# Linear attention before two MLPs: scores and state product in four array tiles of 64 by 64, half of the late scores left out

## What is computed

```python
f = 1.0 / (1.0 + np.exp(-f_logit))
for t in range(S):
    state = f[:, :, t, :, None] * state + np.einsum('bhd,bhe->bhde', k[:, :, t], v[:, :, t])
    y[:, :, t] = np.einsum('bhd,bhde->bhe', q[:, :, t], state)
...
xn = x / rms * rms_g
g = xn @ w_gate
silu = g * (1.0 / (1.0 + np.exp(-g)))
val = xn @ w_val
return (silu * val @ w_out).astype(np.float32)
...
h = x @ w_in
g = np.where(pos, h, np.where(neg, 0.0, (h + beta) ** 2 / (4.0 * beta)))
return (g @ w_out).astype(np.float32)
```

## Time and profile before

| | |
|---|---|
| time, median of 3 runs | 977.84 us (976.65 to 978.01) |
| the profiled execution's own time | 976.92 us |
| its span, first to last instruction | 975.2 us |
| PE busy | 959.0 us (98%), 7651 matmul records |
| DVE busy | 573.8 us (59%) |
| ACT busy | 326.1 us (33%) |
| POOL busy | 22.5 us |
| DMA engines | 12.6% of their time |
| clock granted to PE | 1.0, in all 40 slices |

### The profile page before, as it was taken

One profiled execution on the slowest core, in us unless ns is written; L12 is line 12 of the kernel. 1 busy time (PEld: TensorE's weight loads), 2 busy tenths in 40 slices (PEclk: granted clock), 3 DMA queues, 4 the chain that ended last, 5 costly groups with the idle time before them and its releaser, 6 DMA issues.

```text
span 975.2 us, 19135 instructions
## 1 busy us (share of the span) xinstructions
PE 959.0 (98%) x7651; PEld 868.6 (89%) x7651; DVE 573.8 (59%) x1098; ACT 326.1 (33%) x556; POOL 22.5 (2%) x58
## 2 busy tenths in 40 slices
PE   6899999999999999999999999999999999999998
PEld 5899999999999999999999998888888888888886
DVE  8788666565674765765664665545545455445443
ACT  2433322322322322223223453333333343333333
POOL 0100000000000000000000000000000000000000
PEclk9999999999999999999999999999999999999999
DMA  5541111011111120210111310000000000000000
GB/s 195 181 161 43 41 42 50 32 48 40 40 40 40 40 73 8 72 41 21 60 40 49 122 57 1 1 33 0 0 32 0 0 32 0 32 0 0 32 1 33
DMA packets 16766, 42.32 MB, mean 43 GB/s; under 512 B 1376, under 2 KB 7648, under 8 KB 16736
## 3 DMA queue, kind: packets, MB, share of 16 engines
q1 hardware_dynamic: 16736, 41.88, 12.6%
HBM read 37.16 MB, written 4.72 MB: 43 GB/s over the span
## 4 chain that ended last, share of the span: by engine, by line
PE 94%; DVE 3%; issue 1%; POOL 0%; ACT 0%; DMA 0%; DVEq 0%; POOLq 0%
PE gate_ps L416 15%; PE val_ps L416 15%; PE acc L492 13%; PE gate_ps L480 10%; PE val_ps L480 10%; PE acc L438 10%; PE acc L496 7%; PE acc L442 5%; PE tb L327 2%; PE y_ps L351 2%; PE y_ps L357 2%; PE tb L337 1%; DVE qd L738 1%; PE ta L313 1%; DVE after L717 1%
## 5 line engine op out<-in xcount | busy, mean ns | idle before, releaser
L658 ACT ACTIVATE raw<-raw,half_col 128x512 f32<-128x512 f32 x96 | 69.4, 722 | 155.3 <-DVE raw L909 155.3
L492 PE MATMUL acc<-high,low 128*128 128x512 f32 x285 | 110.9, 389 | 0.0
L492 PE MATMUL acc<-high 128*128 128x512 f32 x285 | 110.9, 389 | 0.0
L597 ACT ACTIVATE act_buf<-gate_ps 128x384 f32<-128x384 f32 x96 | 47.2, 492 | 177.1 <-PE gate_ps L416 177.1
L602 ACT ACTIVATE high<-h_buf 128x384 fp32r<-128x384 f32 x96 | 50.5, 526 | 167.2 <-DVE h_buf L849 167.2
L416 PE MATMUL gate_ps<-high 128*128 (+1 forms) x288 | 99.3, 345 | 1.0 <-issue 0.6
L438 PE MATMUL acc<-high 128*128 128x384 f32 x288 | 99.1, 344 | 0.0
L416 PE MATMUL val_ps<-high 128*128 (+1 forms) x288 | 99.1, 344 | 0.0
L416 PE MATMUL gate_ps<-high,low 128*128 (+1 forms) x288 | 96.5, 335 | 0.0
L416 PE MATMUL val_ps<-high,low 128*128 (+1 forms) x288 | 96.4, 335 | 0.0
L416 PE MATMUL gate_ps<-low,high 128*128 (+1 forms) x288 | 96.4, 335 | 0.0
(11 more groups left out here) (119 smaller groups left out, 1906.8 us busy)
## 6 DMA issues: line engine op xcount, KB each, us to landing
raw<-qkf_dram SPq DMA_DIRECT2D x21, 768.0 KB, 4.3
x_all<-wb_dram SPq DMA_DIRECT2D x12, 576.0 KB, 5.0
v_sb<-v_dram SPq DMA_DIRECT2D x24, 192.0 KB, 2.8
out_dram<-x_all SPq DMA_DIRECT2D x5, 768.0 KB, 3.8
raw<-wc_dram SPq DMA_DIRECT2D x7, 384.0 KB, 3.1
x_all<-qkf_dram SPq DMA_DIRECT2D x2, 768.0 KB, 6.5
kd<-wc_dram SPq DMA_DIRECT2D x3, 384.0 KB, 2.9
qd<-wc_dram SPq DMA_DIRECT2D x3, 384.0 KB, 3.6
```

Of the source, the lines that this page charges most:

```text
L492: pe.matmul(acc[:, m, 0:N2], wc_part(w, j, 1, m), h2_hi[:, j % 2, :], start=(j == 0 and w is w_hi), stop=False)
L658: nc.scalar.activation(act2_buf[:, j % 2, :], act2_buf[:, j % 2, :], ACT.Square, bias=half_col[:, :], scale=0.5).then_inc(square_ready, 1)
```

## The change

- The scores go in four array tiles of 64 rows by 64 columns: for each pair two halves `h` of the keys and two heads `r`. From the fourth chunk on the later 64 keys are multiplied only with the later 64 queries. So that both halves of the array's columns get as much to do, the two key halves stand swapped in the odd pairs (`decay_k` writes them so, in two instructions; `v` comes swapped from the host; the mask has a second form).
- The state product (`recall`) goes in four tiles of 64 by 64 too, one head each, and the state shrinks from 96 to 48 columns. It now stands ahead of `update`, for all four pairs at once, and the values part (`attend`) behind it, also for all pairs.
- `update` goes in strips of 32 and 16 columns, four side by side, the same tiling as `attend`.
- `y_ps` becomes two banks, one for each `r`, and the second is shared with `ta`; the first three chunks use two banks of `acc`. `turn_kd` of later chunks waits for `xs_ready`. In `first_attention` `turn_kd` of the next chunk comes behind the whole `attend`.
- The semaphore `y_made` rises once in a chunk in place of twice, and the weights of the first MLP are reordered on the host to the new order of heads.

```diff
@@ the state, the mask and the banks
-        state = sb("state", [P, 2, NP, 2 * D])
-        decayed = sb("decayed", [P, NP, 2 * D])
+        state = sb("state", [P, 2, NP, D])
+        decayed = sb("decayed", [P, NP, D])
-        causal = sb("causal", [P, C])
+        causal = sb("causal", [P, 2, C])
-        y_ps = bank("y_ps")
-        ta = bank("ta")
+        y_ps = ctx.enter_context(nc.psum_tensor("y_ps", [P, 2, 512], F32))
         tb = bank("tb")
+        ta = y_ps[:, 1, :]
+        y_first = acc[:, 1:3, :]
@@ PE
                 def turn_kd(n, c):
                     pe.wait_ge(kd_ready, n + 1)
-                    if not isinstance(n, int) or n > 0:
+                    if not isinstance(n, int) or n >= CT:
+                        pe.wait_ge(xs_ready, n)
+                    elif n > 0:
                         pe.wait_ge(scores_ready, 2 * n)
...
                     pe.wait_ge(kdT_ready, n + 1)
+                    pe.sem_inc(score_begun, 1)
                     for p in range(NP):
-                        for r, t in enumerate((tb, ta)):
-                            rows = slice(r * HP, (r + 1) * HP)
-                            mm = pe.matmul(t[:, p * C:(p + 1) * C], kd[rows, c % 2, p, :], qd[rows, c % 2, p, :],
-                                           start=True, stop=True)
+                        for h in range(2):
+                            t0 = HP if not first and h != p % 2 else 0
+                            for r, t in enumerate((tb, ta)):
+                                rows = slice(r * HP, (r + 1) * HP)
+                                mm = pe.matmul(t[h * HP:(h + 1) * HP, p * C + t0:(p + 1) * C],
+                                               kd[rows, c % 2, p, h * HP:(h + 1) * HP],
+                                               qd[rows, c % 2, p, t0:C], start=True, stop=True)
                     mm.then_inc(scores_made, 1)
+
+                def recall(n, c, y):
+                    pe.wait_ge(scores_ready, n * 2 + 2)
+                    pe.wait_ge(decayed_ready, n + 1)
+                    if not isinstance(n, int) or n > 0:
+                        pe.wait_ge(xs_ready, n)
+                    pe.sem_inc(recall_begun, 1)
+                    for p in range(NP):
+                        for h in range(2):
+                            q = slice(h * HP, (h + 1) * HP)
+                            for r in range(2):
+                                rows = slice(r * HP, (r + 1) * HP)
+                                pe.matmul(y[q, r, p * D:(p + 1) * D], qd[rows, c % 2, p, q], decayed[rows, p, :],
+                                          start=(p == 0), stop=False, skip_group_check=True)
@@ update(n)
                         for r in range(2):
-                            mm = pe.matmul(tb[r * HP:r * HP + D, p * D:(p + 1) * D], kdT[:, p, r * HP:r * HP + D],
-                                           v_sb[:, r, p, :], start=True, stop=True)
+                            for d0, d1 in ((0, QW), (QW, D)):
+                                rows = slice(r * HP + d0, r * HP + d1)
+                                mm = pe.matmul(tb[rows, p * D:(p + 1) * D], kdT[:, p, rows],
+                                               v_sb[:, r, p, :], start=True, stop=True)
@@ attend
...
+                def attend(n, y):
+                    for p in range(NP):
                         for r in range(2):
                             for s in range(C // QW):
                                 q = slice(s * QW, (s + 1) * QW)
+                                mm = pe.matmul(y[q, r, p * D:(p + 1) * D], scores[:, r, p, q], v_sb[:, r, p, :],
                                                start=False, stop=True, skip_group_check=True)
@@ slot o == 9, and the first chunks
+                            recall(n, c, y_ps)
                             update(n)
-                            attend(n, c, 0)
-                            attend(n, c, 1)
+                            attend(n, y_ps)
...
+                        recall(n, n, y_first)
                         update(n)
-                        attend(n, n, 0)
+                        attend(n, y_first)
                         if n + 1 < CT:
                             turn_kd(n + 1, n + 1)
-                        attend(n, n, 1)
-                        if n + 1 < CT:
                             score(n + 1, n + 1, True)
@@ DVE: decay_k, decay_state, mask_scores
-                    nc.vector.tensor_tensor(kd[:, c % 2, :, :], raw[:, 1, :, :], after[:, :, :], ALU.mult)\
-                        .then_inc(kd_ready, 1)
+                    nc.vector.tensor_tensor(kd[:, c % 2, 0::2, :], raw[:, 1, 0::2, :], after[:, 0::2, :], ALU.mult)
+                    turned, k_odd, after_odd = (x.rearrange("d a (h t) -> d a h t", h=2) for x in
+                                                (kd[:, c % 2, 1::2, :], raw[:, 1, 1::2, :], after[:, 1::2, :]))
+                    nc.vector.tensor_tensor(turned[:, :, ::-1, :], k_odd, after_odd, ALU.mult).then_inc(kd_ready, 1)
...
-                                            whole[:, c % 2, :].unsqueeze(2).to_broadcast([P, NP, 2 * D]), ALU.mult)\
+                                            whole[:, c % 2, :].unsqueeze(2).to_broadcast([P, NP, D]), ALU.mult)\
...
-                                            causal[:, :].unsqueeze(1).to_broadcast([P, NP, C]), ALU.mult)\
+                                            causal[:, :, :].rearrange("p b t -> p (b t)").unsqueeze(1)
+                                            .to_broadcast([P, NP // 2, 2 * C]), ALU.mult)\
```

More of the change, by code:

```diff
@@ L60, with build @@
 SMALLEST = 2.0 ** -60
-def build(nc, qkf, v, rms_g, wb, wc, out, y_rows):
+def build(nc, qkf, v, v_rows, rms_g, wb, wc, out, y_rows):
     ctx = ExitStack()
@@ L157, in build @@
         kdT_ready = sem("kdT_ready")
+        score_begun = sem("score_begun")
+        recall_begun = sem("recall_begun")
         scores_made = sem("scores_made")
@@ L296, in _ @@
                                         base=0, pattern=[[-1, P]], channel_multiplier=1).then_inc(consts_ready, 1)
+                for h in range(2):
+                    rows = slice(h * HP, (h + 1) * HP)
+                    pool.wait_ge(consts_ready, 6 + h)
+                    nc.gpsimd.affine_select(out=causal[rows, 1, :], in_=causal[rows, 1, :], compare_op=ALU.is_ge,
+                                            fill=0.0, base=(h - 1) * HP, pattern=[[1, C]],
+                                            channel_multiplier=-1).then_inc(consts_ready, 1)
                 with pool.Fori(0, NCH) as n:
@@ L387, in keep_warm @@
                     for _ in range(count):
-                        pe.matmul(acc[:, 0, 0:P], ident[:, :], causal[:, :], start=True, stop=True)
+                        pe.matmul(acc[:, 0, 0:P], ident[:, :], causal[:, 0, :], start=True, stop=True)
                 def first_attention():
@@ L778, in update_state, with normalise @@
                     for r in range(2):
-                        rows, cols = slice(r * HP, r * HP + D), slice(r * D, (r + 1) * D)
-                        ins = nc.vector.tensor_tensor(state[rows, 1, :, cols], u[rows, :, :],
-                                                      decayed[rows, :, cols], ALU.add)
+                        rows = slice(r * HP, r * HP + D)
+                        ins = nc.vector.tensor_tensor(state[rows, 1, :, :], u[rows, :, :],
+                                                      decayed[rows, :, :], ALU.add)
                     ins.then_inc(state_ready, 1)
-                def normalise(n):
+                def normalise(n, y=y_ps):
                     dve.wait_ge(rstd_ready, n + 1)
-                    nc.vector.scalar_tensor_tensor(out=xs[:, :], in0=y_ps[:, 0:DM], scalar=rstd[:, :],
-                                                   in1=g_rows[:, :], op0=ALU.mult, op1=ALU.mult)\
+                    heads = [x[:, :].rearrange("t (r m) -> t r m", r=2) for x in (xs, g_rows)]
+                    nc.vector.scalar_tensor_tensor(out=heads[0], in0=y[:, :, 0:NP * D], scalar=rstd[:, :],
+                                                   in1=heads[1], op0=ALU.mult, op1=ALU.mult)\
                         .then_inc(xs_ready, 1)
@@ L957, in _ @@
                         dve.wait_ge(g_loaded, 16)
-                    normalise(n)
+                    normalise(n, y_first)
                 rest_x(0, CT - 1, (gate_ps, val_ps)[(CT - 1) % 2])
@@ L1239 @@
         qkf[:, :, :, :D, a] = x.reshape(B, NP, 2, S // C, C, D).transpose(0, 3, 2, 5, 1, 4)
+    v = v.reshape(B, NP, 2, S // C, C, D).transpose(3, 4, 2, 0, 1, 5)
+    v_turned = v.copy()
+    halves = v.reshape(S // C, 2, HP, 2, B, NP, D)
+    v_turned[:, :, :, :, 1::2] = halves[:, ::-1].reshape(v.shape)[:, :, :, :, 1::2]
+    rows = np.arange(DM).reshape(NP, 2, D).transpose(1, 0, 2).reshape(DM)
     wb = np.stack([
-        moe_w_gate.reshape(KM, P, JB, P).transpose(2, 1, 0, 3),
-        moe_w_val.reshape(KM, P, JB, P).transpose(2, 1, 0, 3),
```

(8 more changed lines are left out.)

54 lines of the change are left out of this document (20 added, 34 removed).

## The result

The changed kernel took 984.29 us (median of 4 runs, 983.25 to 984.56) against 977.87 us of the kernel before on the same chip: ratio 1.0073, 95% interval 1.0060 to 1.0085. It is slower, by 6.4 us; the prediction was 974.2 us and a range up to 978.

What follows compares the result with a forecast made beforehand. PE was taken to bound the loop, DVE the first three chunks. Terms -5.7 - 3.5 + 3.6 + 0.7 + 1.25 = -3.65 us from 976.92 gave 973.3, as a median 974.2 us; range 970.0 to 978.0.

Steps and rivals of the forecast that it cites:

- the slower side: Outcome of a slower changed kernel: chance 0.14, from the quadrants rival and a little of the clock rival.
- Scores, -5.7: Scores on PE in 64 by 64 array tiles: 0.27 us less in each of the loop's 21 chunks.
- State product, update, attend, -0.25 a chunk: These PE products take 1.64 us instead of 1.89; counted in 14 chunks, -3.5 us.
- the first rival: Weight load does not bind: state product records take 0.042 us each, total 971.1 us; chance 0.17.
- The wait at gate(8), +3.6: Late update delays DVE's chain in a tile's chunk 1, so gate(8) starts 0.51 us later, seven times.
- no wait: Rival: something in DVE's chain gives way, so gate(8) does not wait; 968.9 us, chance 0.08.
- decay_k in two, +0.7: DVE's decay_k as two instructions takes 0.1 us more, lying open once in each of seven tiles.
- The first three chunks, +1.25: Before the loop, later updates delay DVE's chain by 1.25 us, ends 0.5 and 2.
- take back 0.85: First three chunks: two shorter decay_state and 0.45 us of DVE idle recover 0.85 us of the delay.
- The clock falls before the loop: Rival: longer PE idle ahead of the first update lowers its clock, costing 1.5 to 3 us; chance 0.07.
- Records strictly in program order: Rival: PE records start in program order, so scores gain half as much, total 976.5 us; chance 0.14.
- the four quadrants share something: Rival: only two of four array tiles run at a time, 25 us more, 999 us; chance 0.12.

Runs made afterwards that it cites:

- e5: Changed kernel, loop kept, with 144 unused semaphore increments among TensorE's products of tile 0, ahead of the loop; 976.60 us.
- e9: Changed kernel, TensorE's loop written out, update first in the first three chunks only, VectorE's second-chunk update_state moved behind use_gate(6) and use_value(6); 967.33 us.
- e7: Changed kernel with TensorE's loop written out and the update ahead of the state product again, in the loop and first three chunks; 971.08 us.
- e4: Changed kernel with its state update in 8 products of 48 columns again instead of 16 of 32 and 16; 989.36 us.
- e12: e9 without the swap of key halves in odd pairs, v in the old order and decay_k one instruction again; 969.98 us.
- e10: e9 with all 128 queries for every half of the keys, so no late key is left out; 971.36 us.
- e11: e9 with TensorE's loop kept as a loop and 130 unused semaphore increments before and behind the first warming products; 982.55 us.
- e6: Kernel before with 192 unused semaphore increments in its loop and 144 more in tile 0, ahead of the loop; 992.8 us.

## Why the prediction was wrong, point by point

**The step that failed** is a term that isn't in the sum: of the 16 more products a chunk the array's time was counted, and their code at nothing. They push the loop body over one block boundary too many, and five jumps cost 8.0 us. It should have been a rival with a price: the order of TensorE's program gives the body's length before and after, and the page of before shows 23 packets of code where a tile takes 1500 instructions, so a body was plainly being kept; what happens when it isn't, no row of before shows. The section of the Trainium skill named above has the size and the warning, and would have given that rival its place. e5 shows that the outcome hung on 144 instructions that do nothing, so nothing in the order of the work could have decided it, and the forecast was also too sure: with that rival the slower side would have held more than 0.14.

**Scores, -5.7: right.** Forecast 0.27 a chunk; measured 0.27, 0.25 and 0.22 in a tile's three chunks, some -5.2 in 21. The timeline of the changed kernel in tile 1, against the earlier trace rows:

```profile
120.56 0.32 PE L341 MATMUL tb<-qd,kd 64*64 64x128 f32 x1
...
120.72 0.27 PE L341 MATMUL tb<-qd,kd 64*64 64x128 f32 x1
...
121.22 0.22 PE L341 MATMUL tb<-qd,kd 64*64 64x64 f32 x1
...
121.39 0.44 PE L435 MATMUL val_ps<-high 128*128 x1
```

From the first record to the next product 0.83 us, 1.09 before. The second record of a tile starts 0.16 behind the first, later long ones take 0.11: the first load was open for 0.05, as forecast, and the step of the shorter records, 0.056 to 0.058, was right too.

**State product, update, attend, -0.25 a chunk: right, a little less.** 0.20 to 0.22 measured. Against the earlier trace rows:

```profile
126.29 0.68 PE L357 MATMUL y_ps<-decayed,qd 64*64 64x48 f32 x32
126.90 0.54 PE L368 MATMUL tb<-v_sb,kdT 128*32 128x48 f32 x32
127.26 0.86 PE L377 MATMUL y_ps<-v_sb,scores 128*32 128x48 f32 x64
128.06 0.45 PE L435 MATMUL val_ps<-high 128*128 x1
```

1.77 us in place of 1.98. Within one array tile the state product's records step 0.058 apart, forecast 0.057, so 64 weight columns do bind over 48 streamed, and the first rival is out.

**The wait at gate(8), +3.6: right.** Timelines of DVE and PE of the changed kernel, against the earlier trace rows; the slot's first record on PE starts at 216.05:

```profile
217.28 0.72 DVE L802 TENSOR_TENSOR state<-tb,decayed 48x192 f32<-48x192 f32 x2 [4.24 <-PE tb L368]
...
218.04 0.56 DVE L866 TENSOR_TENSOR h_buf<-gate_ps,act_buf 128x384 f32<-128x384 f32 x1
...
221.35 0.62 DVE L809 SCALAR_TENSOR_TENSOR xs<-y_ps,rstd,g_rows 128x384 f32<-128x384 f32 x1 [0.45 <-POOL rstd L311]
...
224.56 0.53 DVE L866 TENSOR_TENSOR h_buf<-gate_ps,act_buf 128x384 f32<-128x384 f32 x1
```

`update_state` starts 1.23 behind the slot's start (forecast 1.19) and every link follows at its old distance, but for the 0.07 that the longer `decay_k` adds ahead of 224.56. In tile 1 gate(8) starts 45.97 behind gate(0), 46.10 before, while the chunks ahead of gate(6) had gained 0.65: 0.52 of it is gone, as forecast. Waits of the changed kernel:

```profile
PE gate_ps L435 <- DVE h_buf L866: 4.1, 7, 1.3
```

e9 shows the cause by taking it away: the chain needs `use_gate(6)`, not the update. The rival "no wait" is out.

**decay_k in two, +0.7: right.** The two halves take 415 and 418 ns; gate(2) comes 0.07 later, 0.5 us in seven tiles. So a tile of the loop, jump aside, gained 0.56 where 0.70 was forecast.

**The first three chunks, +1.25: measured 1.6.** The last step came nearly as forecast, the one in the middle didn't. Timeline of DVE, against the earlier trace rows:

```profile
15.46 0.72 DVE L802 TENSOR_TENSOR state<-tb,decayed 48x192 f32<-48x192 f32 x2 [0.66 <-PE tb L368]
...
23.66 0.72 DVE L802 TENSOR_TENSOR state<-tb,decayed 48x192 f32<-48x192 f32 x2 [0.70 <-PE tb L368]
...
27.68 0.62 DVE L809 SCALAR_TENSOR_TENSOR xs<-acc,rstd,g_rows 128x384 f32<-128x384 f32 x1 [0.45 <-POOL rstd L311]
...
30.86 0.72 DVE L802 TENSOR_TENSOR state<-tb,decayed 48x192 f32<-48x192 f32 x2 [1.37 <-PE tb L368]
```

The updates come 0.54, 1.08 and 1.63 later than before (0.7 was forecast for the first). In chunk 2 the update is seen 1.37 behind the second mask, forecast 1.3. The step that failed is "take back 0.85": the 0.45 in which DVE waits for POOL's root is still there at 27.68, since the root moved with the update, and only 0.41 came back, 0.2 from each shorter `decay_state`. The second mask of chunk 2 so ends 0.88 late, forecast 0.55. With the update first (e7, e9) gate(0) is at 35.72 and 35.81.

**Rivals.** *The clock falls before the loop* (0.07) came true beside the forecast's mechanism and cost 1.3 us in the profiled execution, but not from the idle it named. Ahead of the first state product PE idled 2.1 us, forecast 2.4, and the clock stayed at 1.00; it was at 0.50 from 37.69, behind the last `turn_x`, whose idle grew from 1.24 to 2.38. (In e4 it did fall behind the idle that was named, at 15.9.) Nor is such a fall new: of 57 executions of the kernel before beside the experiments, 21 have a mean granted clock of 0.997 or 0.998 and take 976.9 to 978.3 us, the others 976.5 to 977.0. The profiled execution of before is of the second kind, while three of the four times in its median of 977.87 lie where the first kind does. That is why the medians differ by less than the spans, 6.4 against 7.4. The change made a fall that came in a third of the executions one that comes in all of them. *Records strictly in program order* is out (e12), and so is *the four quadrants share something*: in e10 four tiles do all the work of the scores in no more time than two did (gate(2) to gate(3) 5.95 us against 6.00). The rule of the Trainium skill that the prediction weighed (TensorE: Matmul & The Clock Gate, "The mechanism", strict order of starts) does not hold between array tiles here. By the sum's own terms, with the idle of the jumps added, the time would have been 982.2 us, and 983.9 with the clock's 1.3 and the start's 0.35; measured was 984.29.

## What to carry to other kernels

A loop body on TensorE has a size in blocks of code. Count its instructions before and after a change (a small fp32 product is four), look at how many packets the code queue moved, and at the duration of the loop's branch: 0.2 us is a kept body, 3.5 a fetched one. Where it doesn't fit, writing the loop out gave 7.4 us here, and moving it by 144 increments among large products gave 7.7. Increments where PE has no work queued cost more than they gave (e11).

Moving work earlier on the busiest engine moves something later on another: follow the one result that is now late (the update) to the first instruction queued behind its reader. Reordering the reader gave 0.4 us a tile more than undoing the change did.

Skipping work in one column half of the array was worth nothing here until the halves carried equal work (e10 against e12).

## What the runs showed that was not expected

- By the fitted count, TensorE keeps a loop body that lies within 7 blocks of 256 instructions and fetches it anew at 8, whatever its length in between: 1706 instructions free in one place, 1616 not in another. A jump then holds the sequencer for 3.3 to 4.2 us in place of 0.21.
- Semaphore increments on TensorE are free among 128x384 products 0.17 us apart (192 in a tile: 69.16 us against 69.17) and cost 0.15 us each where nothing covers them (e11).
- A tile of the changed kernel takes 0.05 to 0.1 us less as a pass of the loop than written out (68.62 against 68.73, and 67.87 against 67.92). It isn't the keeping: the changed kernel's tile 1, whose code is being fetched, takes 68.63, and the kernel before takes 69.17 either way. Why, no run tells.
- Array tiles of different columns start their records out of the program's order, here by 0.09 us (e12).
- Open: the idle behind a jump varies from 1.1 to 2.4 us, and e6's and e4's are longer than the changed kernel's with a similar branch. How much code lay queued ahead of the branch may be the reason; that wasn't tried.
